# Attention scores computed in plain fp32, two heads at once on the two row halves of TensorE

## The reference

```python
# attention: B=4, H=8, S=576, D=64, blocks of 64
scores = q @ k^T / sqrt(D)
mask   = block_i >= block_j                  # block-causal, blocks of 64
attn   = softmax(where(mask, scores, -1e9))
x      = (attn @ v) as [B*S, H*D]            # 2304 x 512
# dense MLP
h = x @ w_in                                 # 512 x 2048
x = max(0.01*h, h) @ w_out                   # 2048 x 512
# expert layer: tokens with x @ w_skip > 0 go to one of 8 experts
out = x + gate * (relu(x @ w1[e]) @ w2[e])   # 512 x 1024 x 512, other rows: out = x
```

## Time and profile before

| | |
|---|---|
| median of 3 runs | 806.09 us |
| profiled execution | 800.74 us |
| its span, first to last instruction | 798.5 us |
| TensorE busy | 762.1 us, 95% |
| VectorE busy | 381.4 us, 48% |
| ScalarE busy | 308.4 us, 39% |
| GpSimd busy | 165.2 us, 21% |
| mean granted TensorE clock | 0.997 |

### The profile page before, as it was taken

One profiled execution on the slowest core, in us unless ns is written; L12 is line 12 of the kernel. 1 busy time (PEld: TensorE's weight loads), 2 busy tenths in 40 slices (PEclk: granted clock), 3 DMA queues, 4 the chain that ended last, 5 costly groups with the idle time before them and its releaser, 6 DMA issues.

```text
span 798.5 us, 13602 instructions
## 1 busy us (share of the span) xinstructions
PE 762.1 (95%) x4690; PEld 654.8 (82%) x4690; DVE 381.4 (48%) x790; ACT 308.4 (39%) x723; POOL 165.2 (21%) x201
## 2 busy tenths in 40 slices
PE   4887899999999999999999999999999999999997
PEld 3665688888988888899998778787787879999996
DVE  4878555543342464112344555655554341444554
ACT  3656656544443445334342222222321131333533
POOL 5344656321211223200020000000000032222222
PEclk9999999999999999999999999999999999999999
DMA  5646677754544443265766565565652137777750
GB/s 147 169 136 189 180 192 205 205 150 113 140 131 129 126 141 87 75 190 156 191 191 180 159 186 152 169 198 151 180 155 84 54 91 239 241 227 232 232 176 4
DMA packets 101623, 126.84 MB, mean 159 GB/s; under 512 B 15938, under 2 KB 62290, under 8 KB 101560
## 3 DMA queue, kind: packets, MB, share of 16 engines
q1 hardware_dynamic: 98392, 121.37, 52.3%
q0 software_dynamic: 2080, 3.77, 1.5%
q10 hardware_dynamic: 1088, 0.89, 0.5%
HBM read 92.89 MB, written 31.57 MB: 156 GB/s over the span
## 4 chain that ended last, share of the span: by engine, by line
PE 88%; DMA 4%; SPq 4%; issue 1%; ACT 1%; DVE 1%; POOL 0%; POOLq 0%; DVEq 0%; ACTq 0%
PE ps_hid L1612 10%; PE ps_h L1404 9%; PE ps_x L1454 9%; PE ps_x L1456 8%; PE ps_x L1455 8%; PE ps_h L1406 8%; PE ps_h L1405 8%; PE ps_o L1388 5%; PE ps_t L1362 3%; PE ps_y L1624 3%; PE ps_y L1625 3%; PE ps_y L1623 3%; PE ps_s L1347 2%; DMA k<-k_st 2%; PE ps_s L1348 2%
## 5 line engine op out<-in xcount | busy, mean ns | idle before, releaser
L1404 PE MATMUL ps_h<-xh,win_h 128*128 128x384 f32 x384 | 136.4, 355 | 3.0 <-ACT act L891 2.4
L1405 PE MATMUL ps_h<-xl,win_h 128*128 128x384 f32 x384 | 128.8, 336 | 0.0
L1406 PE MATMUL ps_h<-xh,win_l 128*128 128x384 f32 x384 | 128.8, 335 | 0.0
L1454 PE MATMUL ps_x<-wout_h,g_hi 128*128 128x512 f32 x288 | 117.0, 406 | 0.0
L1456 PE MATMUL ps_x<-wout_h,g_lo 128*128 128x512 f32 x288 | 112.5, 391 | 0.0
L1455 PE MATMUL ps_x<-wout_l,g_hi 128*128 128x512 f32 x288 | 112.2, 390 | 0.0
L891 ACT ACTIVATE act<-ps_h 128x384 f32<-128x384 f32 x96 | 47.1, 491 | 151.1 <-PE ps_h L1406 151.1
L1044 DVE COPY pt<-ps_t 128x256 f32<-128x256 f32 (+4 forms) x113 | 49.2, 443 | 107.0 <-PE ps_t L1362 106.8
L1078 DVE TENSOR_TENSOR g_lo<-g_raw,g_hi 128x512 fp32r<-128x512 f32 x72 | 49.6, 688 | 76.0 <-ACT g_hi L901 75.9
L879 ACT ACTIVATE prob<-ps_s,neg_max 128x128 f32<-128x128 f32 (+2 forms) x144 | 78.3, 547 | 9.3 <-DVE neg_max L1038 9.3
L1612 PEld LDWEIGHTS ps_hid<-rows_t,w_sb 128*128 128x128 f32 x704 | 80.2, 192 | 1.7 <-issue 0.8
(11 more groups left out here) (176 smaller groups left out, 1134.9 us busy)
## 6 DMA issues: line engine op xcount, KB each, us to landing
w_sb<-in_w SPq DMA_DIRECT2D x64, 512.0 KB, 5.4
hidden<-act SPq DMA_DIRECT2D x96, 192.0 KB, 2.5
g_raw<-hidden SPq DMA_DIRECT2D x72, 256.0 KB, 4.3
k_raw<-in_k_t SPq DMA_DIRECT2D x62, 144.0 KB, 3.0
q_raw<-in_q_t SPq DMA_DIRECT2D x32, 144.0 KB, 3.2
x2rows<-x SPq DMA_DIRECT2D x18, 256.0 KB, 2.5
out<-x SPq DMA_DIRECT2D x18, 256.0 KB, 2.7
k<-k_st SPq DMA_DIRECT2D x31, 144.0 KB, 2.8
```

The source lines that it names most:

```text
L1404: e.matmul(dst, win_h[:, f, kc, :], xh[slot][:, kc, :], start=kc == 0, stop=False)
L1405: e.matmul(dst, win_h[:, f, kc, :], xl[slot][:, kc, :], start=False, stop=False)
L1406: last = e.matmul(dst, win_l[:, f, kc, :], xh[slot][:, kc, :], start=False, stop=kc == KC - 1)
L1454: e.matmul(dst, hi, wout_h[:, f, :], start=f == 0, stop=False)
```

## The change

q and k of a pair are loaded once, 64 partitions for each head (load_q, load_k), q is scaled in place by VectorE (scale_q), and nothing is split. A query tile of both heads is one group: two plain fp32 matmuls with 64 rows each, on the upper and the lower row half, into two banks, followed by two bf16 matmuls of 64 columns that add the mask. The tail group does the same with 64 rows and 64 columns to a head. A pair has 5 groups; the ring holds two groups. The heads now alternate in the unit order (head_tile), ScalarE's copies stay with the 512-key units (now 7 and 8), p_v of half 0 moves into the pair's own step 7, and o_f has two buffers.

```diff
-            def high_q(n): ...            # ScalarE, 128x640, two a pair
-            def high_k(n): ...            # VectorE, 128x576, two a pair
-            def low_q(n): ...             # VectorE, 64x640, two a pair
-            def low_k(n): ...             # GpSimd, 64x576, two a pair
-            def copy_k(n): ...            # SyncE queue, two a pair
-P_V = {1: (0, 0, 2), 3: (1, 0, 2), 4: (1, 2, 5)}
-PT_ACT = (3, 8)
+P_V = {7: (0, 0, 0, 2), 3: (1, 1, 0, 2), 5: (1, 1, 2, 5)}
+PT_ACT = (7, 8)
+GROUPS = 5
+GROUP_LAST = (1, 3, 4, 6, 8)
+GROUP_AT = {0: 1, 2: 2, 4: 3, 6: 4, 7: 0}
...
+        def load_q(e, p):
+            if p >= 2:
+                e.wait_ge(s_score, GROUPS * (p - 1))
+            e.dma_start(q_sb[p % 2][:, :], pair_in(q_t, p)).then_inc(s_qk[p % 2], 16)
...
+            def scale_q(p):
+                e.wait_ge(s_qk[p % 2], 32 * (p // 2 + 1))
+                e.tensor_scalar(q_sb[p % 2][:, :], q_sb[p % 2][:, :], D ** -0.5, None, ALU.mult).then_inc(s_q, 1)
...
+            def scores(n):
+                p, d = divmod(n, GROUPS)
+                if d == 0:
+                    e.wait_ge(s_q, p + 1)
...
+                if n >= 2:
+                    e.wait_ge(s_exp, UNITS * ((n - 2) // GROUPS) + GROUP_LAST[(n - 2) % GROUPS] + 1)
+                c = 2 * BANK * (n % 2)
+                q, k = q_sb[p % 2], k_sb[p % 2]
+                heads = (slice(0, D), slice(D, P))
+                if GROUP_LAST[d] == TAIL:
+                    for half in range(2):
+                        for own in heads:
+                            last = e.matmul(ps_s[own, c + BANK * half:c + BANK * half + S // 2], q[own, DM:S],
+                                            k[own, S // 2 * half:S // 2 * (half + 1)], start=True, stop=True)
+                    last.then_inc(s_score, 1)
+                    return
+                qt = head_tile(GROUP_LAST[d])[1]
+                cols = P * (qt + 1)
+                for h, own in enumerate(heads):
+                    e.matmul(ps_s[:, c + BANK * h:c + BANK * h + cols], q[own, P * qt:P * qt + P], k[own, 0:cols],
+                             start=True, stop=False)
+                for h, own in enumerate(heads):
+                    last = e.matmul(ps_s[:, c + BANK * h + cols - D:c + BANK * h + cols], mask_q[own, :], mask_k[own, :],
+                                    start=False, stop=True)
+                last.then_inc(s_score, 1)
...
-            scores(1)
             for s in range(STEPS):
-                if s + 2 < N_UNITS:
-                    scores(s + 2)
                 if 2 <= s < N_UNITS + 2:
                     transposes(s - 2)
                 p, i = divmod(s, UNITS)
-                if i in P_V and 1 <= p <= N_PAIRS:
-                    p_v(p - 1, *P_V[i])
-                    if i == 1:
-                        turn_inverse(p - 1)
+                if i == 1 and 1 <= p <= N_PAIRS:
+                    turn_inverse(p - 1)
+                if i in P_V:
+                    back, half, first, end = P_V[i]
+                    if 0 <= p - back < N_PAIRS:
+                        p_v(p - back, half, first, end)
+                if i in GROUP_AT:
+                    n = GROUPS * (p + (i > TAIL + 2)) + GROUP_AT[i]
+                    if n < GROUPS * N_PAIRS:
+                        scores(n)
                 for g, part in FILL[s]:
                     hidden(g, part)
```

More of the change, by code:

```diff
@@ L119, with head_tile, group_of @@
 FILL = fill_steps()
+def head_tile(i):
+    return (i % 2, i // 2) if i < TAIL else ((i - TAIL - 1) % 2, 2 + (i - TAIL - 1) // 2)
+def group_of(u):
+    p, i = divmod(u, UNITS)
+    return GROUPS * p + sum(last < i for last in GROUP_LAST)
 def blocks_of(p):
@@ L183, in build @@
         xl += [sb(f"xl{i}", [P, KC, BLK], F32R, r2) for i in range(2, 4)]
[L184 to L191, removed]
+        q_sb = [sb(f"q_sb{i}", [P, S], F32, r2) for i in range(2)]
+        k_sb = [sb(f"k_sb{i}", [P, S], F32, r2) for i in range(2)]
+        mask_q = sb("mask_q", [P, P], BF16, r2)
+        mask_k = sb("mask_k", [P, D], BF16, r2)
         v_sb = [sb(f"v_sb{i}", [P, QT, P], F32, r2) for i in range(2)]
@@ L195, in build @@
         inv_all = sb("inv_all", [P, S], F32, r2)
-        o_f = sb("o_f", [P, S], F32, r2)
+        o_f = [sb(f"o_f{i}", [P, S], F32, r2) for i in range(2)]
         row_sum = [sb(f"row_sum{i}", [P, UNITS], F32, r2) for i in range(2)]
@@ L307, in build @@
         s_v = [sem(f"s_v{i}") for i in range(2)]
[L308 to L312, removed]
+        s_q = sem("s_q")
         s_score = sem("s_score")
@@ L592, in load_expert @@
                 e.dma_start(dst, src).then_inc(loaded, 16)
[L594 to L600, removed]
+            load_q(e, 0)
+            load_q(e, 1)
+            load_k(e, 1)
             e.dma_start(wg[:, :, :], w_gs).then_inc(s_wg, 16)
@@ L604, in _ @@
                 if p < N_PAIRS:
[L605 to L609, removed]
+                    if i == 1 and 1 <= p < N_PAIRS - 1:
+                        load_q(e, p + 1)
+                        load_k(e, p + 1)
+                    if i == 6 and p + 1 < N_PAIRS:
                         load_v(e, p + 1)
[L611 to L614, removed]
                 if i == 3 and 1 <= p <= N_PAIRS:
@@ L699, in _ @@
             before = [(s_const, N_CONST)]
[L701 to L707, removed]
             def normalise(p):
@@ L1079, in low_g @@
                                 g_hi[j % G_RING][:, :, :].bitcast(F32), ALU.subtract).then_inc(s_glo, 1)
-            high_k(0)
-            e.tensor_copy(k2[0][0:D, :], k_raw[0][0:D, :]).then_inc(s_k2[0], 16)
-            low_q(0)
-            high_k(1)
-            low_q(1)
+            scale_q(0)
             for s in range(STEPS):
@@ L1318, in _ @@
         def _(e):
-            def scores(u):
-                p, i = divmod(u, UNITS)
-                if i in (0, TAIL):
-                    n = 2 * p + (i == TAIL)
-                    e.wait_ge(s_klo, n + 1)
-                    e.wait_ge(s_k2[n % 2], 16 * (n // 2 + 1))
-                    e.wait_ge(s_qlo, n + 1)
-                if u == 0:
-                    e.wait_ge(s_maskd, 32)
-                    e.wait_ge(s_const, N_CONST)
-                if s_freed(u):
-                    e.wait_ge(s_exp, s_freed(u))
-                c = BANK * (s_slot(u) % S_RING)
-                if i == TAIL:
-                    for h in range(2):
-                        for half in range(2):
-                            a, z = S // 2 * half, S // 2 * (half + 1)
-                            dst = ps_s[:, c + BANK * half:c + BANK * half + S // 2]
-                            e.matmul(dst, q_hi[h][:, DM:QW], k_st[h][:, a:z], start=h == 0, stop=False)
-                    for h in range(2):
-                        for half in range(2):
-                            a, z = S // 2 * half, S // 2 * (half + 1)
-                            dst = ps_s[:, c + BANK * half:c + BANK * half + S // 2]
-                            last = e.matmul(dst, q2[h][0:D + 4, DM:QW], k2[h][0:D + 4, a:z], start=False, stop=h == 1)
@@ L1359, in transposes @@
                 if i == TAIL + 1:
-                    e.transpose(t_bank(u, D, P, 2 * P), prob[(u - 1) % P_RING][:, 4 * P:S], ident[:, :])
-                for kt in range(4 if i == TAIL else (i if i < TAIL else i - TAIL - 1) + 1):
+                    e.transpose(t_bank(u, D, 3 * P, 4 * P), prob[(u - 1) % P_RING][:, 4 * P:S], ident[:, :])
+                for kt in range(4 if i == TAIL else head_tile(i)[1] + 1):
                     last = e.transpose(t_bank(u, P, P * kt, P * kt + P), tile[:, P * kt:P * kt + P], ident[:, :])
```

178 lines of the change are left out of this document (47 added, 131 removed).

## The result

The changed kernel takes 794.61 us (794.33 to 794.81, 4 runs) against 805.85 us (803.90 to 807.56, 4 runs): a ratio of 0.986, 95% interval 0.984 to 0.988. That is 11.2 us faster, where I had forecast 9 us slower; it lies near the lower end of the range and near rival 1's 794 us, but not for rival 1's reason.

What follows compares the result with a forecast made beforehand. TensorE was taken to bound the filled stretch, and waits for the copy of k to hold the front. Front -9.6, score product +16.6 and waits +2 gave +9.0 us, added to the median 806.1: 815 us, range 792 to 834.

Steps and rivals of the forecast that it cites:

- rival 1: Row halves of the score matmuls switch shape for free, giving a faster kernel: -12, 794 us; chance 0.30.
- front: Attention from first scores to first woven-in MLP matmul, where engines have slack; period 12.9 us a pair, term -9.6 us.
- filled stretch: Attention from step 50 to 144, 10.4 pairs, where TensorE bounds; the score product was to add +16.6 us.
- step 50: First woven-in MLP matmul, where the front ends; forecast at 80.7 us against 90.25.
- the 3.73 us wait: Longest TensorE wait for the copy of k, before 82.85 us; the lower clock after it was put at 1.7 us.
- The score product: TensorE's score matmuls: 5.1 us a pair against 3.47, so +1.6 a pair and +16.6 us in the filled stretch.
- The step that I called decisive: Entering and leaving the half-array shape costs 0.31 us a block, read from p_v; five blocks a pair, 1.55 us.
- the 2 us for a first pair at the lower clock: Added to the front because the first pair runs on TensorE at the lower clock: 2 us (0 to 4).
- the mechanism of the wait: In the front, two-group ring and ScalarE's queue, high_x included, delay scores: waits of 0.4 and 0.9 us a pair.
- Waits in the filled stretch: TensorE waits longer for ScalarE's copy of a hidden tile, mainly at steps 1 and 8: +2 us (0 to 6).
- Rival 3: In the filled stretch, score groups wait for the newest exponential, 0.4 us each: +21 us, 836 us; chance 0.07.
- Rivals 2: The two heads' score matmuls don't overlap: +3.9 us a pair, +40 in the filled stretch, about 848 us; chance 0.08.

Runs made afterwards that it cites:

- b_again: The kernel before, unchanged, profiled and timed once more: 804.84 us median, ratio 1.000; this profile's span is 805.7 us.
- a_fullrows: New kernel with query tiles' score matmuls on all 128 rows instead of 64: 229.15 us from tail group of pair 6 to that of pair 15, against 218.4.
- a_merged: New kernel with the two p_v blocks of the longer half made into one at step 4: 793.81 us, ratio 0.986 to the kernel before.
- a_highx: New kernel with ScalarE's high_x and GpSimd's low_x moved from steps 0 and 1 to step 2: 792.96 us, ratio 0.984 to the kernel before.
- a_load: New kernel with the splits' load put back on VectorE and ScalarE, on scratch tiles nobody waits for: 800.28 us, ratio 0.990 to the kernel before.
- a_gap: New kernel whose tail group in pairs 1 to 5 also waits for a small DMA: 822.35 us, ratio 1.017 to the kernel before.
- b_busy2: Kernel before with eight small useless matmuls at the head of p_v's half 0 in pairs 0 to 4: 801.20 us, ratio 0.997.

## Why the prediction was wrong

**What bounds the kernel.** Right as a division into front and filled stretch. Wrong in one thing under it: I took 90.25 us as the place of step 50, from one execution whose clock fell once in the front. The median execution is 5 us slower than that one, and b_again shows one where step 50 is at 99.0. The hint was in front of me: the profiled execution stood 5 us under the median, and outside the range, of the runs shown, and I noted that and carried the same 9 us over. I had seen the fall after the 3.73 us wait and priced it at 1.7 us, once. I put 5 of the 11.2 us at the falls that the first profile lacks (the median of before less that execution); with the one that it has it is 6 to 7, and the line through the plain runs gives 6 (805.4 less 799). Both are estimates. The change removes idle stretches that cost more than their own length.

**The score product, +1.6 us a pair.** The step that I called decisive held: full overlap, 0.3 us for each change of shape (0.31 forecast; 0.27 by a_fullrows, 0.31 in a_merged's block), the 512-key group at 1.28 us. The rule of the Trainium skill ("TensorEngine Tiling (Array Packing)", "Key Properties") that a change of tiling mode drains the engine agrees with these for row halves too. (The prediction says there that a free change would be the second rival below; it is the first.) Rival 1, a free change, is refuted, and that its 794 us came out is luck: its filled stretch was to cost +1 us and its front to gain 15. But whole pairs differ by less than the forecast: tail 6 to 15 grew by 10.7 us, 1.19 a pair, or 1.29 without waits (TensorE covered for 204.5 and 216.0 us), in place of 1.6. I had counted five changes of shape of their own in a pair, but the 128-key group stands directly behind a p_v block; from 117.82 to 119.77 in the new kernel the two take 1.45 us, 0.14 less than by my figures. Where the rest goes isn't shown. The term was +16.6 and, with the end and the waits, measured +12.7.

**The front, -9.6 us.** This is the term that failed in size: -18.5 in the first profiles. The first scores came at 5.29 us (7.0 forecast). The period was 12.24, not 12.9: 11.4 us of work where I had 11.8, and 0.8 us of wait where I had 1.3, less 0.2; the mechanism of the wait was right (a_highx). And the 2 us for a first pair at the lower clock did not show: step 50 came 66.4 us after the first scores, where 5.56 periods are 68.1. Matmuls took double for 4 us only, and the first pair, 9.73 us from tail group to tail group, is shorter than the later ones by more than that costs. Together 1.7 + 3.7 + 3.6 = 9.0 us.

**Waits in the filled stretch, +2 us.** Not seen: the wait for the bank is 2.0 us in place of 2.4, and idle time between the tails of pairs 6 and 15 is 2.4 in place of 3.3. Rival 3 with it: no scores wait there at all.

**The sum.** -18.5 + 12.7 = -5.8 by the first profiles, and -27.3 + 14.2 = -13.1 against b_again. Against the median I missed by 20.2 us: 9.0 from the front's length after, 5.9 from the filled stretch (16.6 + 2 forecast, 12.7 measured) and 5.3 from taking one execution's clock before. None of the three alone turns the sign clearly; the front is the largest, and alone would have brought the forecast to about 0. Rivals 2 and 3 are out; a_fullrows shows what lost overlap would cost, and it would have made the kernel slower in the filled stretch.

## What to carry to other kernels

When the profiled execution stands well off the median of the runs, profile again before any sum is made: the part that varies is a cost of the kernel, and a change may remove it. An idle stretch of 2 to 3 us on TensorE is to be priced with what the clock may do behind it, here in the kernel before nothing, 1.7 or 3.4 us more (3.4 or 6.8 us at half speed), and short work put there can be cheaper than none. A matmul on half the rows pays in plain fp32 when both halves run, less some 0.3 us each time the shape changes; put blocks of half-array shape next to each other where nothing waits for the work moved away.

## What the runs showed of the hardware

- The granted clock fell to 0.50 in idle stretches of TensorE of 1.41 (a_load) to 6.0 us (a_gap) or within 2 us behind them, and stayed there for 3.4, 6.8 or 10.2 us, also while TensorE was covered again. Stretches of 1.83 to 2.16 us (the first profile) also passed without a fall; with at most 1.3 us in the front (b_busy2) the profile has none.
- At the start the rows of the granted clock read 1.00 in both kernels, yet matmuls take double: in the new kernel until 9.2 us, 4 us after the first, with pauses of under 0.5 us; before until 22.5 us, 12 us after the first (the prediction has 21.8), with idle stretches of up to 0.8 us among them. What ends it isn't shown.
- Two fp32 matmuls of 64 rows on the two row halves stream 1.64 ns a column together, no more than one alone (1.78). Two half-array blocks directly behind each other shared one change of shape of 0.31 us in a_merged.
